# Token mixing over two batches as seven block products in place of eight

## What is computed

```python
theta = x @ w_theta                           # x: 2 batches x 768 tokens x 512
zr, zi = x * np.cos(theta), x * np.sin(theta)
yr = np.einsum('ts,bsd->btd', w_tok_r, zr)    # w_tok_r, w_tok_i: 768 x 768
yi = np.einsum('ts,bsd->btd', w_tok_i, zi)
u = x + yr + yi
return (u + np.maximum(u @ w_ch, 0.0)).astype(np.float32)
```

## Time and profile before

| | us |
|---|---|
| median of three runs | 527.82 (527.35 to 529.19) |
| the profiled execution | 527.32 |
| its span, first to last instruction | 525.5 |
| PE busy | 520.2 (99%) |
| DVE busy | 249.0 (47%) |
| POOL busy | 191.2 (36%) |
| ACT busy | 167.9 (32%) |
| PE's share of the chain that ended last | 97% |

### The profile page before, as it was taken

How to read it: one execution, slowest core, us unless ns; L and a number is a source line. 1 busy time by engine, 2 the same in 40 slices (tenths; PEclk the granted TensorE clock), 3 DMA queues, 4 the chain that set the end, 5 groups by cost and what they waited for, 6 DMA issues and landing times.

```text
span 525.5 us, 8608 instructions
## 1 busy us (share of the span) xinstructions
PE 520.2 (99%) x3330; PEld 478.5 (91%) x3330; DVE 249.0 (47%) x630; ACT 167.9 (32%) x429; POOL 191.2 (36%) x195
## 2 busy tenths in 40 slices
PE   8999999999999999999999999999999999999997
PEld 7889889988998899989998899898899999999997
DVE  7856647564565352221322213445756388125054
ACT  6645435443453321101112011465654431010010
POOL 6896001010010012991003300132799896462500
PEclk9999999999999999999999999999999999999999
DMA  7873224230220000242000200000022232433102
GB/s 219 276 236 91 65 93 156 85 90 20 71 67 21 1 0 1 80 161 82 0 1 0 91 0 1 0 2 0 3 88 62 61 90 77 135 91 121 30 31 90
DMA packets 24825, 36.65 MB, mean 70 GB/s; under 512 B 2256, under 2 KB 17616, under 8 KB 24784
## 3 DMA queue, kind: packets, MB, share of 16 engines
q1 hardware_dynamic: 24784, 36.09, 21.9%
HBM read 32.94 MB, written 3.15 MB: 69 GB/s over the span
## 4 chain that ended last, share of the span: by engine, by line
PE 97%; POOL 1%; DVE 1%; issue 0%; DMA 0%; ACT 0%; DVEq 0%; POOLq 0%; ACTq 0%
PE bank L1621 19%; PE bank L1012 13%; PE bank L1031 13%; PE bank L1238 13%; PE bank L1256 13%; PE bank L1639 6%; PE bank L1471 6%; PE bank L632 4%; PE bank L572 3%; PE bank L595 3%; POOL bias L443 1%; PE bank L1481 1%; PE bank L919 1%; PE bank L541 1%; PE bank L992 1%; PE bank L610 1%
## 5 line engine op out<-in xcount | busy, mean ns | idle before, releaser
L1012 PE MATMUL bank<-xnT,w1h 128*128 128x256 f32 x368 | 69.6, 289 | 0.0
L1238 PE MATMUL bank<-xnT,w1h 128*128 128x384 f32 x256 | 65.2, 335 | 0.0
L1621 PE MATMUL bank<-ring_h,z_hi 128*128 128x384 f32 x192 | 64.6, 337 | 0.0
L1621 PE MATMUL bank<-ring_h,z_lo 128*128 128x384 f32 x192 | 64.2, 334 | 0.0
L1621 PE MATMUL bank<-ring_l,z_hi 128*128 128x384 f32 x192 | 64.1, 334 | 0.0
L1012 PEld LDWEIGHTS bank<-xnT,w1h 128*128 128x128 f32 x368 | 57.3, 191 | 2.2 <-issue 1.8
L1383 POOL TENSOR_TENSOR trig<-x,trig 128x512 f32<-128x512 f32 x24 | 32.5, 1376 | 66.6 <-ACT trig L1430 66.6
L1012 PE MATMUL bank<-xnT,w1l 128*128 128x256 f32 x184 | 51.9, 282 | 0.0
L907 POOL TENSOR_SCALAR rtmp<-mean_var 128x2 f32<-128x2 f32 x6 | 1.6, 272 | 129.2 <-DVE mean_var L879 129.2
L1238 PEld LDWEIGHTS bank<-xnT,w1h 128*128 128x128 f32 x256 | 46.4, 188 | 0.6
L1366 POOL TENSOR_TENSOR ring_l<-raw,ring_h 128x768 fp32r<-128x768 f32 x24 | 46.1, 1921 | 2.0
(11 more groups left out here) (136 smaller groups left out, 1117.3 us busy)
## 6 DMA issues: line engine op xcount, KB each, us to landing
raw<-wtokT SPq DMA_DIRECT2D x24, 384.0 KB, 3.3
raw<-w SPq DMA_DIRECT2D x7, 1024.0 KB, 6.4
v_sb<-vwin SPq DMA_DIRECT2D x16, 256.0 KB, 2.8
q_sb<-qT SPq DMA_DIRECT2D x24, 128.0 KB, 3.7
outT<-out_sb SPq DMA_DIRECT2D x16, 192.0 KB, 1.9
k_sb<-kcols SPq DMA_DIRECT2D x16, 184.0 KB, 3.7
v_sb<-vwin SPq DMA_DIRECT2D x8, 192.0 KB, 4.1
k_sb<-kcols SPq DMA_DIRECT2D x8, 132.0 KB, 3.8
```

The costliest lines, as they stand in the source:

```text
L1012: last = nc.tensor.matmul(bank_of(n)[:, 0:AN], wt[q][:, d, f * P:(f + 1) * P], xnT[:, AT * c:AT * c + AT, low, d, :], start=d == 0 and m = ...
L1238: last = nc.tensor.matmul(h_bank[f % 2][:, 0:CN], wt[slot][:, d, fs], tokens(low, d), start=first, stop=(d == DC - 1 and wt is w1l))
L1621: last = nc.tensor.matmul(bank, zt[b][:, s, r, ds], wt[j % RING][:, r, :], start=(s == 0 and r == 0 and m == 0), stop=(s == TILES - 1 and ...
```

## The change

The eight block products become seven (P1 to P7, a form of Strassen's scheme), of sums and differences of the blocks of z and of the weights:

- PRODUCTS = 7, in the order P1, P2, P6, P5, P7, P3, P4. Each has six steps of 4 x 3 = 12 matmuls of 384 columns (line 1829 of the changed kernel), so a step is half as long as before: 504 matmuls in place of 576. P1, P6, P7 and P4 accumulate in banks 2 to 5 without being cleared; P2 has banks 6, 7, 0 and 1, and then P5 and P3 together.
- After each product DVE adds the banks into the transposed x in place (add_product, line 1735, 2 or 3 instructions for each channel block). A product may not write its banks before the product two earlier has been added (y_added).
- Blocks of z: z of both batches stays in SBUF unsplit. z_hi and z_lo of batch 0 are made as before and serve P1 and P2. For batch 1 DVE makes, for each tile, three differences (sums, lines 1587, 1591 and 1593), and later a sum (first_sum, 1746), 512 elements each. For P6, P5, P7, P3 and P4, ACT makes the high part of a step's z (1563) and DVE the low part (sum_low_part, 1580), 512 elements.
- Blocks of weights: each piece is 384 elements. For P1 and P2 POOL splits them (1450, 1453) as before. P6 needs three pieces from HBM and two differences, one on DVE (tok_difference, 1742) and one on POOL (1475); P7 and P4 need one difference each on POOL (1478, 1482). Their high parts are made by ACT (1575), their low parts by POOL (1487). The ring has six places.
- DMA: the pieces of 192 KB number 6 for P1, 6 for P2, 18 for P6, none for P5, 12 for P7, 6 for P3 and 6 for P4; SP waits for the end of the rotation before those of P6.
- The four channels stages all stand behind P4 on PE. u is split straight from the transposed x, in 2 or 3 instructions for each channel block (1709 on ACT, 1754 on DVE); the low part of w_ch moves from DVE to POOL, behind all of its low parts (1515); the output is formed from PSUM and x in one pass of 2 or 3 instructions (1766).

```diff
-            for n in range(len(MIX)):
-                mix(n)
-                if n >= 1:
-                    channels(n - 1)
-            channels(len(MIX) - 1)
+            for n in range(PRODUCTS):
+                product(n)
+            for k in range(len(CHANNELS)):
+                channels(k)
...
-                        for r in range(2):
-                            for m, (zt, wt) in enumerate(((z_hi, ring_h), (z_hi, ring_l), (z_lo, ring_h))):
+                        for m, (zt, wt) in enumerate(((z_hi, ring_h), (z_hi, ring_l), (z_lo, ring_h))):
...
+            def tok_sums(j):
+                n, s = divmod(j, TILES)
+                if n == P6:
+                    pool.wait_ge(t1_ready, s + 1)
+                    nc.gpsimd.tensor_tensor(w_t2[s][:, :], w_t2[s][:, :], w_t1[s][:, :], ALU.subtract).then_inc(tok_sum, 1)
+                elif n == P7:
...
+            tok_sums(P6 * TILES)
+            for j in range(P6 * TILES, STEPS):
+                n, s = divmod(j, TILES)
+                if j + 1 < STEPS:
+                    tok_sums(j + 1)
+                tok_low(j)
+            pool.wait_ge(ch_hi, 1)
+            nc.gpsimd.tensor_tensor(wcl[:, :, :], raw_ch, wch[:, :, :].bitcast(F32), ALU.subtract).then_inc(ch_split, 1)
...
+            def first_sum(s):
+                nc.vector.tensor_tensor(z[1][s][:, 0, :], z[1][s][:, 0, :], z[1][s][:, 1, :], ALU.add).then_inc(s1_ready, 1)
...
             for t in range(TILES + 1, TT + 3):
                 rotation_vector(dve, t)
+                if t >= TILES + 3:
+                    s = t - TILES - 3
+                    sums(dve, s)
+                    if s >= 1:
+                        sum_low_part(dve, P6 * TILES + s - 1)
+            sum_low_part(dve, P6 * TILES + TILES - 1)
+            for s in range(2):
+                tok_difference(s)
+            add_product(P1)
+            for s in range(2, TILES):
+                tok_difference(s)
+            for s in range(TILES):
+                first_sum(s)
+            add_product(P2)
+            for n in (P5, P7, P3, P4):
+                for s in range(TILES):
+                    sum_low_part(dve, n * TILES + s)
+                if n < P3:
+                    add_product(n - 1)
+                if n == P5:
+                    u_lows(0)
+                if n == P3:
+                    add_product(P7)
+            add_product(P3)
+            u_lows(1)
+            add_product(P4)
+            for k in range(len(CHANNELS)):
+                outputs(k)
+                if k + 2 < len(CHANNELS):
+                    u_lows(k + 2)
```

More of the change, by code:

```diff
@@ new lines, in tok_high_part, with sum_low_part @@
+        def tok_high_part(act, j):
+            n, s = divmod(j, TILES)
+            if n in (P6, P5):
+                act.wait_ge(tok_sum, s + 1)
+            elif n in SUMMED:
+                act.wait_ge(tok_sum, sums_done(j))
+            else:
+                act.wait_ge(tok_loaded[j % TILES], tok_count(j))
+            wait_used(act, j - RING)
+            nc.scalar.activation(ring_h[j % RING][:, :], tok_of(j), ACT.Copy).then_inc(tok_high, 1)
+        def sum_low_part(dve, j):
+            dve.wait_ge(sum_high, j - P6 * TILES + 1)
+            nc.vector.tensor_tensor(z_slot(z_lo, j), z_of(j), z_slot(z_hi, j).bitcast(F32),
+                                    ALU.subtract).then_inc(sum_split, 1)
@@ L1535, in mixing_scalar, with u_highs @@
                 rotation_scalar(act, t)
-            act.wait_ge(z_split, TT)
+                if t >= TILES + 4:
+                    sum_high_part(act, P6 * TILES + t - TILES - 4)
+            sum_high_part(act, P6 * TILES + 4)
+            sum_high_part(act, P6 * TILES + 5)
+            for s in range(TILES):
+                tok_high_part(act, P6 * TILES + s)
+            def u_highs(k):
+                b, th = CHANNELS[k]
+                if k == 1:
+                    act.wait_ge(tok_split, (P7 + 1) * TILES)
+                if k >= 2:
+                    act.wait_ge(v_mm, (k - 1) * DC)
+                for d in range(DC):
+                    act.wait_ge(y_added, last_added(k) * DC + d + 1)
+                    for home, cols in x2T_parts(b, th, d):
+                        last = nc.scalar.activation(uTh[:, k % 2, d, cols], home, ACT.Copy)
+                    last.then_inc(u_high, 1)
@@ L1537, in mixing_scalar @@
+            for j in range(P5 * TILES, STEPS):
+                if j == P7 * TILES:
+                    u_highs(0)
+                sum_high_part(act, j)
+                tok_high_part(act, j)
+            act.wait_ge(sum_split, (P3 - P6 + 1) * TILES)
             act.wait_ge(ch_loaded, 16)
             nc.scalar.activation(wch[:, :, :], raw_ch, ACT.Copy).then_inc(ch_hi, 1)
-            for k in range(len(MIX) * DC):
-                th, d = MIX[k // DC][1], k % DC
-                act.wait_ge(u_added, CT * (k + 1))
-                if k >= HALVES * DC:
-                    act.wait_ge(out_ready, k - HALVES * DC + DC - d)
-                nc.scalar.activation(uTh[:, th, d, :], u_sum[:, k % 2, :], ACT.Copy).then_inc(u_high, 1)
```

306 lines of the change are left out of this document (205 added, 101 removed).

## The result

| | before | changed |
|---|---|---|
| median, us | 527.59 (527.35 to 529.19, 4 runs) | 535.51 (535.05 to 537.17, 4 runs) |
| ratio to before | | 1.0149, interval 1.0119 to 1.018 |
| span of the profiled execution | 525.5 | 534.0 |
| PE busy | 520.2 (99%) | 515.1 (96%) |
| DVE, POOL, ACT busy | 249.0, 191.2, 168 | 300.7, 206.0, 192.8 |

A forecast was written before the change was run, and what follows sets the result against it. PE bound the kernel before; after the change, DVE and POOL taking turns at the SBUF port make it wait. 527.32 - 12.48 + 20.6 of waits + 0.1 + 2 for the clock = 537.5, stated as 537.0 us; range 529 to 543.

The forecast's parts named there:

- the rival in which the clock stays: Whole kernel: DVE's and POOL's queues make PE wait, but PE's clock does not fall; 535.5 us, chance 0.25.
- 72 matmuls less: PE, block products: 504 matmuls in place of 576, at 0.1733 us each, save 12.48 us.
- (a) rotation: Rotation steps 10 to 12: DVE and POOL both need more than PE's 5.29 us a step; PE waits 2.8 us.
- (b) P2: P2: POOL's split with two DVE holds takes 2.5 us a step against 2.08, and POOL comes late; waits 2.4 us.
- (c) P6, first step: Start of P6: differences on DVE and POOL, then the first low part, make PE wait 4.2 us.
- (c) P6, inside: Later P6 steps: POOL's two instructions with DVE holds take 2.97 us against 2.08, four times; PE waits 3.6 us.
- (d) P7: Before P7: a DVE chain of 23.7 us against about 16.1 us of PE; PE waits 7.6 us.
- clock behind it: After the wait before P7: PE's clock falls to 1.2 GHz for one step, 2 us; bounds 0 and 8.3.
- The pace of PE and the shares of DVE and POOL: Before the change: 0.1733 us per 384-column matmul; between 374 and 400 POOL busy 25.58 of 26.00 us, DVE 14.63.
- The price of a turn: SBUF port: DVE's 512 and POOL's 384 in turn take 0.53 + 0.95 = 1.48 us, against 0.60 for DVE alone.
- What would show it: PE some 95% busy, four places of 2 to 8 us waits, longest before P7; z_lo near 1.5, POOL's 384 near 1.2.
- the port does not bind: Rival, whole kernel: DVE and POOL share the port without turns, only P6's start waits, about 0.5; 515.3 us, chance 0.08.

The follow-up runs named there:

- e5: Changed kernel with u_lows(0)'s twelve instructions reading unused PSUM columns instead of the transposed x in SBUF; 526.51 us.
- e2: Changed kernel with the weights' differences and low parts of P6 to P4 moved from POOL to DVE (48 instructions of 384 elements); 528.32 us.
- e3: Changed kernel with 18 filler matmuls for PE before P6 and 50 before P7, begun as a new sum in bank 2; 537.66 us.
- e7: Changed kernel with 8 filler matmuls before P6 and 26 before P7, which leave the bank's sums standing; 534.67 us.
- e4: e2 with DVE's and ACT's queues reordered by need (adding P1 and P6's first step before the last two rotations' sums, u_lows(0) behind add_product(P5)); 523.05 us.
- e6: Changed kernel with POOL's differences for P6 and P7 cut to 8 of 384 elements; 529.28 us.
- e8: e6 with add_product(P2) moved ahead of the six first sums on DVE; 525.42 us.
- e9: e4 with 2 filler matmuls before P6's first step and 7 before its second; 522.78 us.

## Why the prediction was right, step by step

The median of 535.51 lies 1.5 under the 537.0, and the signs and places held. The number alone would not decide: it is also, to 0.1, the 535.5 of the rival in which the clock stays, and only the traces tell the two apart. That rival's sum came close because the waits were sized too long (20.6 forecast, 18.0 measured) by about what the clock then took; in the forecast itself the two errors, 2.6 too much and 0.8 too little, partly cancel. The terms, each measured as the excess of the starts of two steps over 2.08 or 5.29 us:

| term | forecast | measured |
|---|---|---|
| 72 matmuls less | -12.5 | -12.5 |
| (a) rotation | 2.8 | 2.7 |
| (b) P2 | 2.4 | 1.4 |
| (c) P6, first step | 4.2 | 4.1 |
| (c) P6, inside | 3.6 | 3.2 |
| (d) P7 | 7.6 | 6.6 |
| clock behind it | 2 | 2.8 |

The measured waits and the clock sum to 20.8, and 525.5 - 12.5 + 20.8 = 533.8 stands against the span of 534.0.

**The pace of PE and the shares of DVE and POOL** came out of the rows as taken; P7 and P4 to the last output hold no wait, the loads of P6 never end a wait, and wcl on POOL (488.22 to 492.84) leaves 4.8 us before the channels, 4 forecast.

**The price of a turn** was a little high: 1.42 in place of 1.48, which leaves 0.45 for DVE's 512 beside POOL's 0.97 in place of 0.53. A u_low beside POOL is 1.02 from start to start, not 1.08. In (d) the DVE chain of 23.7 us was 22.95 (2.37 + 8.13 + 2.12 + 9.55 + 0.78); it began 0.42 after P6's fifth step (433.89), not with its last as I had it. So PE had eight steps in front of it, 16.93, and no wait in P5, where I had counted seven steps and 1.5 of waiting, 16.1; that these come out near each other is luck. 22.95 + 0.42 - 16.93 = 6.44. In (b) I let POOL come later out of the rotation than it did: the first step that waits (P2's fourth) waited 0.9, not 1.6, the next two 0.25 each.

**The clock** was the step with no row behind it; one step's worth, 2, was too low for P7, where two steps took 3.98 and 2.99 us. Its fall before P6 (0.50 from 422.2 to 425.6) I had not priced; it lies inside the waits that POOL's pace sets in P6, and inside the 3.2.

**What would show it**, as forecast: PE at 96%, the longest wait before P7, uTl of 128 at 0.85 to 1.09 us in their groups, POOL's 384 at 1.26. The mean of the z_lo of 512 is 1.08, not near 1.5: the forecast price holds where POOL is busy (1.36 from start to start in P5, 1.42 for the first sums), and in P7 and P3 POOL idles for long parts.

**The rivals.** That the port does not bind falls with e5, where only the place of an input changes and 9.0 us come back, and with e2. That the clock stays falls with the window 457 to 463 and with e3 and e7. The fall was not worse than forecast by more than 1.

The removed matmuls did give their 12.5 us; e4 shows 4.5 of them left once DVE and POOL stop taking turns in front of PE.

## What to carry to other kernels

A product fewer on PE pays only what the sums around it leave over. Before moving elementwise work onto both DVE and POOL, count their instructions with all inputs in SBUF as one queue; one DVE with the work of both was faster here by 7.2 us (e2), and one input read from PSUM by 9.0 (e5, with a wrong operand in its place, so only as a measure). Put in DVE's queue what PE needs next ahead of what it needs later, and fill a wait of several us with small matmuls only where the feeder is ahead again behind it.

## What was not expected of the hardware

- DVE and POOL do not share the port evenly. In most places they alternate, 1.42 us for a 512 and a 384; but behind an unbroken run of DVE instructions with both inputs in SBUF POOL waited 5.00 us (e6, for 8 elements) and 4.56 us (e8). In no timeline here, from 360 us on, does DVE wait for more than one POOL instruction. The Trainium skill ("SBUF — State Buffer", section "SBUF: two separate sides") has an exclusive lock for a whole instruction, which goes to the side that starts first. The runs agree on the whole instruction, and add that several of one side can pass in a row. On who starts first they are less clear: in e8 POOL's record starts 0.02 us ahead and still ends last.
- The granted clock fell to 0.5 after waits of 0.68 and 1.81 us close together (e4, until 429.7), as it did in single waits of 3.81 and 6.44. But waits of 2.73, 1.22 and 1.38 passed without a fall (e8, clock 1.00 up to PE's end); what decides is open. How much of a fall costs time depends on the feeder: 2.7 to 3.0 us before P7, 0.3 by the medians in e4 against e9.
- A filler of identity by identity in fp32 is two PE instructions and takes 0.22 us (11.16 us for 50, 5.80 for 26). Begun as a new sum in columns that nobody reads, it drops the unfinished sums in the other columns of its bank: the output of e3 is off by 0.49 (relative error), and that of e7, whose fillers add to what stands there, is not.
